# State product of a delta-rule attention on 64x64 quarters of the array, one key product bank, and weights loaded in twelve pieces

## The reference

```python
for t in range(S):
    kt, vt, bt = (k_n[:, :, t], v[:, :, t], beta[:, :, t, None])
    y[:, :, t] = np.einsum('bhd,bhde->bhe', q[:, :, t], state)
    v_old = np.einsum('bhde,bhd->bhe', state, kt)
    state = state + bt[:, :, :, None] * np.einsum('bhd,bhe->bhde', kt, vt - v_old)
...
h = x @ w_in                       # 3072 x 384 @ 384 x 2048
g = np.where(h > 0.0, h, np.exp(np.minimum(h, 0.0)) - 1.0)
x = g @ w_out
...
for e in range(E):                 # each token goes to its 2 best experts
    out[mask] += top2_w[mask, k, None] * (np.maximum(x[mask] @ w1[e], 0.0) @ w2[e])
```

## Time and profile before

| what | value |
|---|---|
| median of 3 runs | 1184.32 us (1182.23 to 1185.56) |
| the profiled execution | 1183.98 us |
| its span | 1182.2 us |
| PE busy | 1133.9 us (96%), 11596 matmul records |
| DVE, ACT, POOL busy | 646.2, 462.6, 355.9 us |
| mean granted TensorE clock | 0.993 |
| the chain that ended last | PE 73% of the span, all of it behind the attention loop |

### The profile page before, as it was taken

The page is one execution under the profiler, slowest core; times in us unless marked ns, Lnnn a source line. Parts: engine busy times, 40 slices in busy tenths (PEclk is TensorE's granted clock), DMA queues, the critical chain, the costliest instruction groups (busy, mean ns, idle before and its releaser), DMA issues.

```text
span 1182.2 us, 29103 instructions
## 1 busy us (share of the span) xinstructions
PE 1133.9 (96%) x11596; PEld 1079.6 (91%) x11596; DVE 646.2 (55%) x1552; ACT 462.6 (39%) x1048; POOL 355.9 (30%) x378
## 2 busy tenths in 40 slices
PE   5898899898999999999999999999999999999996
PEld 3896788677999999999999999999999999999995
DVE  4968877663456556564655657522535353434442
ACT  1236565576343333333333335422424333333331
POOL 4299696244000120210202012322222222323223
PEclk9999999899999999999999999999999999999998
DMA  7543545943999110111101011472424242424221
GB/s 157 137 122 72 119 96 135 300 109 78 397 362 309 60 42 20 41 40 40 41 20 41 1 63 61 172 228 65 170 64 170 64 173 74 172 85 159 64 71 52
DMA packets 81962, 137.29 MB, mean 116 GB/s; under 512 B 10922, under 2 KB 69906, under 8 KB 80570
## 3 DMA queue, kind: packets, MB, share of 16 engines
q1 hardware_dynamic: 67850, 87.97, 25.4%
q0 software_dynamic: 12992, 28.75, 7.7%
q10 hardware_dynamic: 1008, 18.97, 4.3%
HBM read 81.96 MB, written 53.77 MB: 115 GB/s over the span
## 4 chain that ended last, share of the span: by engine, by line
PE 73%; DVE 1%; issue 0%; ACT 0%; POOL 0%; ACTq 0%; POOLq 0%
PE ps_x L1385 18%; PE ps_x L1475 18%; PE ps_h L1374 17%; PE ps_h L1453 17%; PE ps_r L1433 2%; PE ps_r L1424 1%; DVE hg L1793 0%; ACT hg L1583 0%; POOL out_dram L1340 0%; DVE w_parts L1756 0%; PE ps_r L1492 0%; DVE x_raw L1786 0%; PE ps_r L1402 0%; ACT yT_d L1601 0%; PE ps_r L1400 0%
## 5 line engine op out<-in xcount | busy, mean ns | idle before, releaser
L1475 PE MATMUL ps_x<-hg,w_parts 128*128 128x400 f32 x1152 | 230.2, 346 | 0.0
L1385 PE MATMUL ps_x<-w_parts,hg 128*128 128x400 f32 x1152 | 229.7, 345 | 0.0
L1374 PE MATMUL ps_h<-xg,w_parts 128*128 128x384 f32 x1152 | 222.3, 338 | 0.0
L1453 PE MATMUL ps_h<-xg,w_parts 128*128 128x400 f32 x1116 | 220.5, 345 | 1.1 <-DVE w_parts L1756 1.1
L1385 PEld LDWEIGHTS ps_x<-w_parts,hg 128*128 128x128 f32 x1152 | 209.6, 188 | 0.0
L1793 DVE SCALAR_TENSOR_TENSOR hg<-ps_h,hg 128x400 fp32r<-128x400 f32 x128 | 73.5, 574 | 243.3 <-ACT hg L1583 242.8
L1374 PEld LDWEIGHTS ps_h<-xg,w_parts 128*128 128x128 f32 x1152 | 204.0, 188 | 2.5 <-DVE elu_parts L1650 2.5
L1453 PEld LDWEIGHTS ps_h<-xg,w_parts 128*128 128x128 f32 x1116 | 202.7, 188 | 4.0 <-issue 3.1
L1475 PEld LDWEIGHTS ps_x<-hg,w_parts 128*128 128x128 f32 x1152 | 206.0, 188 | 0.0
L1320 POOL DMA_INDIRECT xs_scratch<-x,rows_now x48 | 49.5, 1031 | 393.2 <-DVE rows_now L1730 294.1
L1583 ACT ACTIVATE hg<-ps_h 128x400 fp32r<-128x400 f32 x128 | 64.7, 505 | 256.3 <-PE ps_h L1453 256.3
(11 more groups left out here) (175 smaller groups left out, 1326.8 us busy)
## 6 DMA issues: line engine op xcount, KB each, us to landing
xs_scratch<-pads SPq DMA_DIRECT2D x2, 5502.0 KB, 42.0
x_rows<-xs_scratch SPq DMA_DIRECT2D x17, 614.1 KB
kqT<-in_kqT_dram SPq DMA_DIRECT2D x48, 192.0 KB, 3.8
carried<-in_w_dram ACTq DMA_DIRECT2D x3, 3072.0 KB, 11.7
w_raw<-in_w_dram ACTq DMA_DIRECT2D x3, 3072.0 KB, 11.4
xs_scratch<-pads SPq DMA_DIRECT2D x6, 1375.5 KB, 17.0
inversion<-in_w_io_dram SPq DMA_DIRECT2D x4, 1536.0 KB, 12.9
out_dram<-pads SPq DMA_DIRECT2D x1, 4800.0 KB, 29.3
```

The lines of the kernel that those rows point to most:

```text
L1374: mm = nc.tensor.matmul(ps_h[f % 2][:, 0:TB], wi[:, a, k, f * P:(f + 1) * P], xr[:, b, k, :], start=(i == 0), stop=(i == len(passes) - 1))
L1385: mm = nc.tensor.matmul(ps_x[t][:, 0:DG], act_r[:, f % RING, a, t * P:(t + 1) * P], wo[:, b, f, :], start=(f == 0 and i == 0), stop=(f == ...
L1453: mm = nc.tensor.matmul(ps_h[f % 2][:, 0:TR], w1, xg[:, b, k, :], start=(m == 0), stop=(m == len(passes) - 1))
L1475: mm = nc.tensor.matmul(ps_y[k][:, 0:TR], w2r[i][:, a, s, k * P:(k + 1) * P], hg[:, s % RING, b, :], start=(s == 0 and m == 0), stop=(s == ...
```

## The change

- `outputs(n)`: the state's part contracts over each head's own 48 rows. Four products (two pairs p, two heads h) go to the four 64x64 quarters: head h on row half h, its output on column half h for even p and 1 - h for odd p. Even p write PSUM bank 4, odd p bank 5. Then the four full-height products of x follow, then the same again for the other two pairs.
- To have the second bank, `ps_k` is one bank instead of two. So `keys_on_state(n)` waits until `right_side(n - 1)` has read it.
- The copy of the outputs (`take_outputs`) reads two banks and restores the order of pairs. Heads of odd pairs have changed sides, so a chunk is stored with four DMAs, not two.
- `ps_wo` is one bank, `ps_gate` another. `turn_output_weights(f)` waits for ACT's copy of tile f - 1, not f - 2, and `gate_columns(f - 1)` follows it.
- The weights come in 12 DMAs of about 0.5 MB, three in each of m = 7 to 10: one behind each store of the iteration and one at its end.
- Set 4 of group 2 is transposed before the loop, set 5 and the squares at m = 0, and the norms are taken at m = 1, not 2. The memset of the outputs' bank covers both banks.

```diff
+        ps_p, ps_g = ([psum[:, i + j] for j in range(2)] for i in (2, 6))
+        ps_y = psum[:, 4:6, 0:2 * P].rearrange("p b (q t) -> p b q t", t=P)
+        ps_k, ps_s = psum[:, 0], psum[:, 1]
+        ps_wo, ps_gate = psum[:, 6, 0:D], psum[:, 7]
...
+        def output_rows(p, h):
+            return slice(PADH * (h ^ p % 2), PADH * (h ^ p % 2) + DH)
...
             def store(n):
-                for h in range(2):
...
+                for b in range(2):
+                    for h in range(2):
+                        sp.dma_start(xt_dram.rearrange("(q e d) t -> e d q t", e=4, d=DH)[2 * b + h, :, :, at:at + C],
+                                     yT[n % 2][output_rows(b, h)].rearrange("d (q b) t -> d q b t", b=2)[:, :, b]
+                                     ).then_inc(outputs_stored[n % 2], 16)
...
+                pieces = [(m - W_PAIR + 1) * W_EACH + i for i in range(W_EACH)] if W_PAIR - 1 <= m < PAIRS - 1 else []
                 for n in (2 * m - 2, 2 * m - 1):
                     if m:
                         store(n)
+                        for i in pieces[n % 2:n % 2 + 1]:
+                            load_weights(i)
...
-                    for i in range(W_LOADS):
-                        load_weights(i)
+                for i in pieces[2:]:
+                    load_weights(i)
...
             def keys_on_state(n):
-                if n >= B + 2:
-                    pe.wait_ge(rhs_ready[n % 2], (n - B) // 2)
+                if n > B:
+                    pe.wait_ge(rhs_ready[(n - 1) % 2], (n - 1 - B) // 2 + 1)
...
             def turn_output_weights(f):
-                if f >= 2:
-                    pe.wait_ge(wo_turned_sb, f - 1)
+                if f:
+                    pe.wait_ge(wo_turned_sb, f)
...
             def outputs(n):
-                for p in range(NP):
-                    for h in range(2 if n >= B else 0):
-                        nc.tensor.matmul(ps_y[heads(h), p * P:(p + 1) * P], state[n % B][:, p, h * DH:(h + 1) * DH],
-                                         kqT[n % DEEP][:, p // QP, 1, p % QP, :], start=True, stop=False)
-                    for h in range(2):
-                        mm = nc.tensor.matmul(ps_y[heads(h), p * P:(p + 1) * P], x[n % KEPT][:, 2 * p + h, :],
+                for q in range(NP // 2):
+                    four = [(p, h) for p in (2 * q, 2 * q + 1) for h in range(2)]
+                    for p, h in four if n >= B else ():
+                        nc.tensor.matmul(ps_y[output_rows(p, h), p % 2, q], state[n % B][heads(h), p, h * DH:(h + 1) * DH],
+                                         kqT[n % DEEP][heads(h), p // QP, 1, p % QP, :], start=True, stop=False)
+                    for p, h in four:
+                        mm = nc.tensor.matmul(ps_y[output_rows(p, h), p % 2, q], x[n % KEPT][:, 2 * p + h, :],
                                               lq[n % KEPT][:, 2 * p + h, 1, :], start=(n < B), stop=True)
...
             # DVE
-            nc.vector.memset(ps_y, 0.0).then_inc(y_cleared, 1)
+            nc.vector.memset(psum[:, 4:6], 0.0).then_inc(y_cleared, 1)
+            to_set_lanes(2, (4,))
...
-                if m == 2:
+                if m == 1:
                     take_norms(2)
                     turn_norms(2)
...
-                if m < 2:
-                    to_set_lanes(2, (4 + m,))
-                if m == 1:
+                if m == 0:
+                    to_set_lanes(2, (5,))
                     square_norms(2)
```

More of the change, by code:

```diff
@@ L282, in store @@
                 at = (n // B + n % B * NCH) * C
-                for h in range(2):
-                    sp.dma_start(xt_dram.rearrange("(p h d) t -> h d p t", h=2, d=DH)[h, :, :, at:at + C], yT[n % 2][heads(h)]
-                                 ).then_inc(outputs_stored[n % 2], 16)
+                for b in range(2):
[3 more added lines that the diff above has]
+                                     ).then_inc(outputs_stored[n % 2], 16)
             def load_weights(i):
-                at, size = W_CUTS[i * W_EACH], WI_COLS // 2
-                to, given = w_raw[:, at:W_CUTS[(i + 1) * W_EACH]], w_io[:, i * size:(i + 1) * size]
-                if i >= W_LOADS // 2:
+                at, to = W_CUTS[i], w_raw[:, W_CUTS[i]:W_CUTS[i + 1]]
+                if at < WI_COLS:
+                    given = w_io[:, at:W_CUTS[i + 1]]
+                else:
                     to = to.rearrange("p (f d) -> p f d", d=DG)[:, :, 0:D]
-                    given = given.rearrange("p (f d) -> p f d", d=D)
+                    at = WI_COLS + (at - WI_COLS) // DG * D
+                    given = w_io[:, at:at + to.shape[1] * D].rearrange("p (f d) -> p f d", d=D)
+                if i == 0:
+                    for p in range(2):
+                        sp.wait_ge(inv_placed[p], W_PAIR * NR)
+                if i == W_EACH:
+                    sp.wait_ge(from_lanes, NSET)
                 sp.dma_start(to, given).then_inc(w_loaded[i], 16)
@@ L726, in take_turned @@
                     act.wait_ge(gate_done, f - 1)
[L727 removed]
+                nc.scalar.activation(wo_turned[:, f % 2].rearrange("p k t -> p (k t)"), ps_wo, ACT.Copy
                                      ).then_inc(wo_turned_sb, 1)
@@ L731, in take_gate @@
                 act.wait_ge(gate_done, FT1)
-                nc.scalar.activation(gate.rearrange("p (c b e) -> p b c e", b=2, e=GATES),
-                                     ps_gate.rearrange("p b (c e) -> p b c e", e=GATES), ACT.Copy).then_inc(gate_taken, 1)
+                nc.scalar.activation(gate, ps_gate[:, 0:FT1 * GATES], ACT.Copy).then_inc(gate_taken, 1)
             def set_gate():
```

39 lines of the change are left out of this document (14 added, 25 removed).

## The result

The changed kernel takes **1188.29 us** in the median (1186.22 to 1193.21, 11 runs) where the kernel before, beside it, takes 1183.44 us (1182.23 to 1185.56, 11 runs). The ratio is 1.0044, with a 95% interval of 1.0033 to 1.0055: 4.85 us slower. The forecast was 1183.8 us and no change, so it missed by 4.5 us; the time lies in the range. The profiled execution of after took 1186.89 us (span 1185.1 us), 1.4 us under its median.

The account below looks back on a forecast made before the run. PE bounds the kernel, its queue setting undisturbed passes, with late instruction fetches disturbing passes 7 to 9. Terms -4.9 - 0.7 + 0.1 + 2.7 + 1.6 + 0.9 = -0.3 us gave 1183.8 us, range 1178.0 to 1190.0.

Parts of the forecast that it names:

- The first step that failed: Norms moved to m = 1: the wait for DVE only moves, waits at the start of m = 2 go; -0.7 us.
- The second: Weights in twelve pieces, passes 7 to 9: of 5.9 us winnable, 1.0 us stays lost; -4.9 us (-2 to -6).
- A piece of 0.5 MB fills the engines for some 1.5 us: Weight loads: at 360 GB/s, three times a pass; a fetch can still fall into one, so 1.0 us stays.
- The key bank: keys_on_state waits about 0.5 us for right_side, delaying each pass 0.3 us; +2.7 us over m = 1 to 10.
- The quarters: State's part of outputs: overlap wins 0.44 us a chunk, changes of shape cost 0.53 us; +1.6 us over 18 chunks.
- Quarters and stores together: Outputs' state part (+1.6 us) and the last store's two extra issues at the loop's end (+0.1 us).
- Before the loop: Tile 1 waits about 0.8 us for ACT's copy of tile 0 in a chain without slack; +0.9 us (0 to 2).
- Small pieces disturb as much: Rival: half the pieces' gain goes, longer waits bring low clock, 0.5 us wait each pass; 1189.6 us, chance 0.20.
- Its own test: Deciding sign of the small-pieces rival: one PE wait over a microsecond in m = 8 or 9 that "issue" ends.
- Changes of shape are cheap: Rival: half the 0.53 us shape cost in outputs goes, pieces gain their full 5.9 us; 1178.6 us, chance 0.28.
- in turns: Rival: two row halves can't write one PSUM bank, so each chunk's outputs lose 0.53 us; 1191.7 us, chance 0.08.
- The signs that the prediction gave: Passes 3 to 6 up 0.3 to 0.6 us; 216 to 255 us: no issue wait over 0.6 us; passes 8, 9 below 16.5.

Follow-up runs that it names:

- e10: Kernel before with one key bank and its wait, set 4 before the loop, set 5 and squares at m = 0, norms at m = 1: +5.0 us, ratio 1.0050.
- e17: Changed kernel with four large weight loads and the part before the loop undone: +7.5 us against the kernel before, ratio 1.0061.
- e11: Changed kernel with the weights in four large loads again, the rest kept: +7.8 us against the kernel before, ratio 1.0075.
- e5: Kernel before with only the lanes moved (set 4, set 5, squares) and the norms at m = 1: +0.4 us, ratio 1.0005.
- e4: Kernel before with only one bank for the keys' product and its wait: +3.0 us, ratio 1.0024.
- e8: Changed kernel with POOL held back at m = 1 until the norms are taken: +5.8 us against the kernel before, ratio 1.0044.
- e1: Changed kernel with the norms back at m = 2, lanes and squares still early: +6.1 us against the kernel before, ratio 1.0050.
- e3: Kernel before with only the twelve weight pieces: +1.1 us, ratio 1.0002.
- e6: Kernel before with only the part before the loop changed (one bank for turned tiles, another for the gate): -0.2 us, ratio 0.9995.
- e7: Kernel before loading an eighth of the weights' bytes, outputs of layers 2 and 3 not the reference's: -5.9 us, ratio 0.9954.
- e2: Changed kernel with the state's part of the outputs over all 128 rows again: +6.4 us against the kernel before, ratio 1.0054.
- e12: Changed kernel with set 5, squares and norms of group 2 ahead of the loop: +5.7 us against the kernel before, ratio 1.0044.
- e13: Changed kernel loading an eighth or less of the weights' bytes: +2.2 us against the kernel before, ratio 1.0023.
- e16: Changed kernel with the part before the loop undone: +5.0 us against the kernel before, ratio 1.0042.
- e14: Changed kernel with norms ahead of the loop and an eighth of the weights' bytes: +1.7 us against the kernel before, ratio 1.0019.
- e15: Kernel before with one key bank, lanes and norms at m = 1, and twelve weight pieces: +5.6 us, ratio 1.0056.

## Why the prediction was wrong, by its own steps

By the pairs of runs the difference is made up of key bank and norms +5.0 (e10), quarters and stores +2.5 (e17 less e10), the part before the loop +0.4 (e11 less e17) and the pieces -3.0 (after less e11), which gives 4.9. The sum comes out by construction, since each part is the difference of two neighbours in one chain of kernels (before, e10, e17, e11, after). By the ratios the same parts are +5.9, +1.3, +1.7 and -3.7 us, and only the first and the last are clear of zero. The forecast of the same parts was 2.0, 1.7, 0.9 and -4.9. So of the 5 us that the sum was off, some 3 lie in key bank and norms and some 2 in the pieces; these are the two steps that failed.

- **The first step that failed: "the same DVE work at m = 1 stands at the same place of the pass, so this loss moves and doesn't shrink".** It grew. At m = 1 POOL still eliminates group 1, and the steps of the norms last 2.0 us longer beside it. I had looked at what POOL waits for, and not at what it does beside DVE. The term was -0.7 us; alone it measured +0.4 us (e5), and beside the key bank +2.0 us (e10 less e4, not clear of the noise). Key bank and norms together were forecast at -0.7 + 2.7 = 2.0 us and measured 5.0 us (3.9 to 7.8 by the ratio, so the excess over 2.0 is clear of the noise). The timed runs put the loss on the pair, and the trace shows the longer steps in it; that they are the whole of the missing 3 us isn't shown, since e8 and e1 took them away and gained nothing. The low clock doesn't explain it either. The prediction had one more stretch of it in a rival, at 1.8 us. It lasts 6.8 us in after and 3.4 us in the kernel before, but also 6.8 us at m = 2 of e3 and e6, which leave the norms as they were, and 3.4 us in e8.
- **The second: the pieces, -4.9 forecast, nothing alone (ratio 1.0002, at best -1.3 us) and -2.4 to -3.0 us in company.** In company each pair alone is too noisy to exclude -4.9; alone it is excluded. What could be won was sized right (5.9 us, e7). The 1.0 us that the sum left in place was not. "A piece of 0.5 MB fills the engines for some 1.5 us" took the rate of full engines for the time in which a piece can delay a fetch; a piece lands 5.6 us behind its issue, and in the 85 us of the DMA view the pieces alone raise the engines' time from 0.548 x 85 x 16 = 745 us for 13.36 MB to 0.593 x 85 x 16 = 806 us for 13.27 MB (e3). So twelve pieces reach over more places of the instruction stream: e3's third wait at 257 us is one that the large loads don't have.
- **The key bank: +2.7 forecast, +3.0 measured.** Right in mechanism and size: 0.56 us of waiting and 0.40 us a pass, where 0.5 and 0.3 stood; the wait at m = 7 is 2.51 us, where 2.5 stood.
- **The quarters: +1.6 forecast.** The mechanism was right (the quarters overlap, each change costs a gap) and the size 0.09 us a chunk too high: 1.88 us before and after. That the quarters take turns is ruled out by 0.36 us for four products. (By itself had shown less than the prediction read from it: 1.01 us lies between the 1.31 us of two at a time and 0.65 us, 3 x 0.218, of four.)
- **Quarters and stores together: +1.7 forecast, +2.5 us with large loads (e17 less e10), which isn't clear of the noise.** Outputs have no part in it, and no run has the quarters or the four stores alone. Behind the first outputs of m = 12, 0.54 us are lost where 0.1 stood. They stand in one wait of PE, between its last outputs and the next layer's first product. It is 0.96 us in all nine kernels with two stores a chunk and 1.36 to 1.79 us in all ten with four (1.45 in after, where SP's issues of the last eight stores reach to 294.74 us and PE goes on at 295.19 us). Pass 6 takes 16.9 to 17.7 us in the kernels with four stores (after, e2, e8, e11, e12, e13, e16, e17; but 16.3 in e1 and 16.1 in e14), in all of these but e8 with an instruction wait of 0.4 to 1.2 us like that of 188.37 us, and 16.1 to 16.4 in e4, e10 and e15. What brings it is open.
- **Before the loop: +0.9 forecast; -0.2 alone, +0.4 (e11 less e17) and -0.2 (after less e16) in company.** None is a measurable cost: ACT's copy that PE now waits for is covered. In e16 the first solve does start at 85.19 us, where after starts it at 86.37, but the time stays at 1188.6 us.
- **The rivals.** "Small pieces disturb as much" gave 1189.6 us and came nearest, with three marks: 0.4 us a pass for the key bank instead of 0.3, a low clock at the long wait of m = 1, and pieces that gained too little. Its own test, one instruction wait of more than a microsecond in m = 8 or 9, is met in e3 (1.27 and 1.21 us), not in the profile of after (0.81 us). So the number is near partly by luck. "Changes of shape are cheap" fell with the 1.88 us, "in turns" with the 0.36 us.
- **The signs that the prediction gave.** Several spoke against it: pass 6 is 2.0 us longer than 15.68 us, where +0.3 to +0.6 stood, and an instruction wait of 0.81 us stands between 216 and 255 us, where none over 0.6 was to be. Pass 8, at 16.94 us, is over its 16.5 as well. And the sum, from 1183.7 us with medians 0.3 us higher, gives 1184.0 and not 1183.8 us, which changes nothing.

## What to carry to other kernels

Before work is moved on an in-order engine, read what the neighbour engine does in the new place, not only who waits there; and then time the move together with the waits that stand behind it, and not only by itself. Splitting a large load doesn't shorten the time in which it can delay something else, and may lengthen it; its worth was nothing alone and 3 us in the whole change, so it has to be timed in both. A stall which stands at fixed places of the instruction stream moves with every edit, so an edit's gain in one pass can be taken back in a later one: judge by timed medians with a bare run of each part, and of the pairs that share a wait, and don't read a gain of a few microseconds off one profile.

## What the runs showed of the hardware

- **PE's instructions come through the DMA engines.** Queue q8 brings 15 packets in 85 us, and each of PE's 53 instruction waits of over 0.45 us between 150 and 300 us ends 1.2 to 1.6 us behind the end of such a packet. They last up to 2.65 us when the weights' bytes are on the way; with an eighth of the bytes none over 0.3 us is left behind 195 us. The Trainium skill, Runtime: NRT & Kernel Launch, section "Instruction fetch mechanics", tells of refills in blocks of 16 KiB by a DMA queue of the engine's own, which the trace's packets of 16384 bytes agree with; it calls the cost mostly hidden, and here the measurement decides: 5.9 us in passes 7 to 11 of the kernel before weren't.
- **Small DVE steps stretched up to fourfold beside POOL.** Three float32 steps of 64 columns took 0.84 to 0.87 us beside POOL's products of 0.80 to 0.86 us and 0.19 to 0.23 us without them (e8). Not every step did: two others of the same group, at 111.93 and 114.67 us, took 0.34 and 0.23 us beside POOL. The Trainium skill, SBUF — State Buffer, section "Who interferes with whom", has an exclusive lock on a port pair shared by the two; it names instructions with two inputs in SBUF, and some with one, as those that meet it, and that a step of 0.84 us lasts as long as POOL's instruction beside it agrees with that.
- **Two row halves of the array wrote one PSUM bank at once**, each its own partitions: four products of 128 columns took 0.36 us with the change of shape behind them, where two took 0.218 us before. The 0.14 us between is what one change costs in the earlier trace rows (0.09 to 0.15 us), so the four ran in the time of two.
